# Queries and keys that arrive head dimension first, split for two heads at once, and three small row operations on GpSimd

## What is computed

```python
# q, k, v: [2, 8, 768, 64] float32 (16 heads of 768 tokens), proj: [64, 6]
q_bits = (q @ proj > 0); k_bits = (k @ proj > 0)
q_bucket = sum(q_bits * 2**arange(6)); k_bucket likewise
scores = where(q_bucket[:, None] == k_bucket[None, :], q @ k.T / 8, -1e9)
attn = exp(scores - max(scores)); attn = attn / (sum(attn) + 1e-9)
attn_out = attn @ v            # then x [1536, 512] goes through two mixtures of 8 experts
```

## Time and profile before

| what | value |
|---|---|
| median of three runs | 1698.58 us |
| profiled execution, from first to last instruction | 1694.0 us |
| TensorE, VectorE, ScalarE, GpSimd busy over the span | 94%, 40%, 30%, 18% |
| start of the first exponential | 19.24 us |
| first transposes of attention's output for the expert layer | 304.22 us |
| the same four engines, 150 to 185 us (two heads) | 34.15, 32.91, 28.33, 13.28 of 35.00 us |

### The profile page before, as it was taken

One profiled execution on the slowest core, in us unless ns is written; L12 is line 12 of the kernel. 1 busy time (PEld: TensorE's weight loads), 2 busy tenths in 40 slices (PEclk: granted clock), 3 DMA queues, 4 the chain that ended last, 5 costly groups with the idle time before them and its releaser, 6 DMA issues.

```text
span 1694.0 us, 21627 instructions
## 1 busy us (share of the span) xinstructions
PE 1591.6 (94%) x7588; PEld 1310.1 (77%) x7589; DVE 670.9 (40%) x1227; ACT 505.0 (30%) x943; POOL 309.6 (18%) x381
## 2 busy tenths in 40 slices
PE   7999998789999999999999999999999992699997
PEld 6888887568888888888888888888888871577775
DVE  6999998541211211211221121121122134554324
ACT  5887877301111111111111111111111133643213
POOL 3333341320030030030030030030030004322202
PEclk9999999999999999999999999999999995899999
DMA  5343343110110110020020020010011013753310
GB/s 136 92 119 93 104 124 123 51 50 1 50 50 1 50 50 0 15 84 0 0 99 0 0 99 0 0 65 34 0 50 50 1 50 131 271 176 133 134 43 23
DMA packets 49380, 108.06 MB, mean 64 GB/s; under 512 B 7350, under 2 KB 13494, under 8 KB 49344
## 3 DMA queue, kind: packets, MB, share of 16 engines
q1 hardware_dynamic: 44208, 96.30, 17.3%
q10 hardware_dynamic: 2736, 4.98, 1.0%
q0 software_dynamic: 2400, 6.31, 1.0%
HBM read 81.58 MB, written 13.40 MB: 56 GB/s over the span
## 4 chain that ended last, share of the span: by engine, by line
PE 80%; DVE 7%; issue 5%; ACT 3%; DMA 3%; POOL 2%; DVEq 0%; ACTq 0%; POOLq 0%; SPq 0%
PE psum L353 24%; PE psum L355 23%; PE psum L354 23%; PE psum L576 2%; DVE pt_lo L1069 2%; DMA w_raw<-in_moe_w_dram 2%; DVE row_max L1079 1%; PE psum L528 1%; ACT prob L846 1%; PE psum L784 1%; PE psum L565 1%; ACT pt_hi L839 1%; PE psum L566 1%; PE psum L589 1%; PE psum L590 1%
## 5 line engine op out<-in xcount | busy, mean ns | idle before, releaser
L936 ACT ACTIVATE h_hi<-psum 128x512 fp32r<-128x512 f32 x192 | 114.9, 599 | 871.8 <-PE psum L355 871.8
L353 PE MATMUL psum<-xt_lo,w_hi 128*128 128x512 f32 x768 | 304.8, 397 | 0.0
L355 PE MATMUL psum<-xt_hi,w_lo 128*128 128x512 f32 x768 | 301.6, 393 | 0.0
L353 PE MATMUL psum<-w_lo,h_hi 128*128 128x512 f32 x768 | 299.5, 390 | 1.6 <-issue 1.6
L354 PE MATMUL psum<-xt_hi,w_hi 128*128 128x512 f32 x768 | 299.4, 390 | 0.0
L355 PE MATMUL psum<-w_hi,h_lo 128*128 128x512 f32 x768 | 299.1, 390 | 0.0
L354 PE MATMUL psum<-w_hi,h_hi 128*128 128x512 f32 x768 | 298.8, 389 | 0.0
L1232 DVE SCALAR_TENSOR_TENSOR h_lo<-psum,h_hi 128x512 fp32r<-128x512 f32 x192 | 132.7, 691 | 347.9 <-ACT h_hi L936 347.5
L1262 DVE SCALAR_TENSOR_TENSOR tok<-psum,route,tok 128x512 f32<-128x512 f32 x96 | 65.7, 745 | 436.4 <-PE psum L355 436.4
L379 POOL CAST w_hi<-w_raw 128x512 fp32r<-128x512 f32 x64 | 39.2, 612 | 813.4 <-PE psum L355 813.4
L355 PEld LDWEIGHTS psum<-xt_hi,w_lo 128*128 128x128 f32 x768 | 144.6, 188 | 33.8
(11 more groups left out here) (227 smaller groups left out, 2020.5 us busy)
## 6 DMA issues: line engine op xcount, KB each, us to landing
...
```

The source lines that it names most:

```text
L353: pe.matmul(acc, a[0], b[1], start=start, stop=False)
L355: return pe.matmul(acc, a[1], b[0], start=False, stop=stop)
L936: act.activation(h_s[0][:, f, :], psum[:, f % 4, :], ACT.Relu).then_inc(m1.h_hi, 1)
```

## The change

Queries and keys are laid out otherwise on the host, before the kernel is launched: two heads lie on one another, head dimension first, as [8 pairs, 128, 768]. The kernel loads a pair with two transfers of 384 KB each and splits it into `k_hi`, `k_lo`, `q_hi` and `q_lo` (128 x 768), once for two heads. The transposes of keys and queries and the ScalarE copies behind them are gone. Instead SP moves all six operands of a head from the split tiles, where it moved four before. The hash of half a head has five matmuls: two of them use 64 partitions (`k_lo` against the high and low part of the projection), and one takes both parts of the projection against `k_hi` twice (`proj_mix`). It stands in r1 and r2, one step later than before. The turned outputs are no longer transposed and then added by GpSimd: a float32 matmul with `fold` (two unit matrices on one another, 128x64) turns and adds at once, so that ScalarE copies 192 columns and GpSimd only scales. `row_scale`, `row_bias` and the denominator move from VectorE to GpSimd, which now follows the same steps: row terms of tile g+2 first, then pieces of a split. The reciprocal stays on VectorE, in r1 and r4.

The core of the diff:

```diff
         gate_in = w_gate.rearrange("(k p) e -> p k e", p=P)
+        def load_pair(i):
+
+            sp.wait_ge(s_qk_split, 2 * i)
+            sp.sem_inc(s_load_go, 1)
+            sp.dma_start(k_raw[:], k[i]).then_inc(s_k_in, 16)
+            sp.dma_start(q_raw[:], q[i]).then_inc(s_q_in, 16)
+
...
+        def move(i, u, first=False):
+
+
+            rows = slice(u * D, u * D + D)
+            k_split, q_split, scored = 2 * i + 1, 2 * i + 2, IT * (2 * i + u - 1)
+            sp.wait_ge(s_qk_split, k_split)
+            if not first:
+                sp.sem_inc(s_load_go, 1)
+                sp.wait_ge(s_sc, scored)
+            for dst, src in ((k_hh[u][0:D, :], k_hi), (k_hh[u][D:P, :], k_hi), (k_b[u][0:D, :], k_lo)):
+                sp.dma_start(dst.bitcast(F32), src[rows, :].bitcast(F32)).then_inc(s_moved[u], 16)
+            sp.wait_ge(s_qk_split, q_split)
+            for dst, src in ((q_t[u][0:D, :], q_hi), (q_t[u][D:P, :], q_lo), (q_b[u][0:D, :], q_hi)):
+                sp.dma_start(dst.bitcast(F32), src[rows, :].bitcast(F32)).then_inc(s_moved[u], 16)
+
+        def move_bits(i, u):
+
+            sp.wait_ge(s_bits, 2 * (2 * i + u) + 2)
+            sp.dma_start(k_b[u][HQ:HK, :].bitcast(F32), q_b[u][HK:P, :].bitcast(F32)).then_inc(s_bk[u], 16)
+
+        def pair(i, last=False):
+            move(i, 0)
+            load_v(2 * i + 1, 1)
+            if not last:
+                load_pair(i + 1)
+            move_bits(i, 0)
+            move(i, 1)
+            if not last:
+                load_v(2 * i + 2, 0)
+            move_bits(i, 1)
...
-        load(0, 0)
+        for u in range(2):
+            sp.dma_start(v_raw[u][:].rearrange("p t d -> p (t d)"), v_v[u]).then_inc(s_v_in[u], 16)
+        for u in range(2):
+            sp.wait_ge(s_k_b, u + 1)
+            move(0, u, first=True)
+        load_pair(1)
         sp.dma_start(gate_raw[:], gate_in).then_inc(s_setup_dma, 16)
         sp.dma_start(one_col[:, 0:1], tau.partition_broadcast(P)).then_inc(s_setup_dma, 16)
...
+        move_bits(0, 0)
+        load_v(2, 0)
+        move_bits(0, 1)
+        sp.wait_ge(s_zeros, 1)
+        with sp.Fori(1, NH // 2 - 1) as it:
+            pair(it)
+            fill(it - 1)
+        pair(NH // 2 - 1, last=True)
+        fill(NH // 2 - 2)
...
+        def split_qk(i, r):
+
+            if r == 0:
+                pool.wait_ge(s_moved[1], 96 * i)
+                pool.wait_ge(s_k_in, 16 * i + 16)
+                copy(k_hi[:], k_raw[:]).then_inc(s_qk_hi, 1)
+            if r in (1, 2):
+                a = slice((r - 1) * HALF, r * HALF)
+                pool.wait_ge(s_qk_hi, 2 * i + 1)
+                sub = pool.tensor_tensor(k_lo[:, a], k_raw[:, a], k_hi[:, a].bitcast(F32), ALU.subtract)
+                if r == 2:
+                    sub.then_inc(s_qk_split, 1)
+                    pool.wait_ge(s_q_in, 16 * i + 16)
+                    copy(q_hi[:], q_raw[:]).then_inc(s_qk_hi, 1)
+            if r == 3:
+                pool.wait_ge(s_qk_hi, 2 * i + 2)
+                pool.tensor_tensor(q_lo[:], q_raw[:], q_hi[:].bitcast(F32), ALU.subtract).then_inc(s_qk_split, 1)
...
+        def row_terms(it, u, t):
+
+            g = IT * (2 * it + u) + t
+            c = slice(t % 2, t % 2 + 1)
+            pool.wait_ge(s_max, g + 1)
+            pool.sem_inc(s_pool_go, 1)
+            pool.tensor_scalar(row_scale[:, c], row_max[:, c], -BIG / 2, SCALE, ALU.is_gt, ALU.mult).then_inc(s_scale, 1)
+            pool.wait_ge(s_scale, g + 1)
+            pool.sem_inc(s_pool_go, 1)
+            pool.tensor_scalar(row_bias[:, c], row_max[:, c], row_scale[:, c], -1.0, ALU.mult,
+                               ALU.mult).then_inc(s_bias, 1)
+
...
+        def step(it, kk):
+            g = 2 * IT * it + kk
+            if known(it, g + 2):
+                row_terms(*at_step(it, kk, 2))
+            if kk % 3 == 0 and known(it, g - 3):
+                i, u, t = at_step(it, kk, -3)
+                denominators(i, u, t // 3)
+            if kk % 3 == 1 and known(it, g - 7):
+                i, u, t = at_step(it, kk, -7)
+                tail(i, u, t // 3)
+            i, r = divmod(kk, 2 * IT)
+            if r < 4 and known(it, 2 * IT * (it + i + 1)):
+                split_qk(it + i + 1, r)
+            if kk % IT == IT - 1 and known(it, g + 1):
+                i, u = divmod(kk // IT + 1, 2)
+                split_v(it + i, u, first=isinstance(g, int) and g < IT)
...
-                    mm = pe.matmul(psum[:, bank, 0:HALF], w[part][:], src[:, half * HALF:(half + 1) * HALF],
-                                   start=(w is proj_w[0] and part == 1), stop=(w is proj_w[1] and part == 0))
+            a = slice(half * HALF, (half + 1) * HALF)
+            o = psum[:, bank, 0:HALF]
+            if half == 0:
+                pe.wait_ge(s_moved[u], 96 * it + 96)
+            for part in (1, 0):
+                pe.matmul(o, proj_w[0][part][:], q_t[u][:, a], start=(part == 1), stop=False)
+                pe.matmul(o, proj_w[1][part][0:D, :], k_b[u][0:D, a], start=False, stop=False)
+            mm = pe.matmul(o, proj_mix[:], k_hh[u][:, a], start=False, stop=True)
             mm.then_inc(s_proj, 1)
...
-                tr = pe.transpose(psum[:, 7, j * P:(j + 1) * P], o_t[:, j * P:(j + 1) * P], ident[:])
-            tr.then_inc(s_o_nat, 1)
+                mm = pe.matmul(psum[:, 7, j * D:(j + 1) * D], o_t[:, j * P:(j + 1) * P], fold[:], start=True, stop=True)
+            mm.then_inc(s_o_nat, 1)
...
-                    pe.wait_ge(*((s_qk_ready, 4 * n + 8) if kk % IT == 0 else (s_bits, 2 * n + 4)))
+                pe.wait_ge(s_bits, 2 * (n + kk % IT // 3) + 2 if known(it, IT * (n + kk % IT // 3)) else 2 * NH)
                 turn_outputs(it, kk)
...
+        for part in range(2):
+            rows = slice(part * D, part * D + D)
+            link(dve.tensor_copy(proj_mix[rows, :], proj_w[1][part][rows, :].bitcast(F32)))
...
-        dve.wait_ge(s_raw[0], 48)
-        for rows, raw in ((k_s[0], k_raw[0]), (q_s[0], q_raw[0])):
-            link(dve.tensor_copy(rows[:, :, 0:D].bitcast(F32R), raw[:]))
-            dve.tensor_tensor(rows[:, :, D:2 * D].bitcast(F32R), raw[:], rows[:, :, 0:D],
-                              ALU.subtract).then_inc(s_qk_split, 1)
+        dve.wait_ge(s_k_in, 16)
+        dve.tensor_copy(k_hi[:], k_raw[:]).then_inc(s_qk_hi, 1)
+        dve.wait_ge(s_qk_hi, 2)
+        dve.tensor_tensor(k_lo[:], k_raw[:], k_hi[:].bitcast(F32), ALU.subtract).then_inc(s_qk_split, 1)
+        dve.tensor_tensor(q_lo[:], q_raw[:], q_hi[:].bitcast(F32), ALU.subtract).then_inc(s_qk_split, 1)
...
-            dve.wait_ge(s_max, g + 1)
-
-            dve.tensor_scalar(row_scale[:, c], row_max[:, c], -BIG / 2, SCALE, ALU.is_gt, ALU.mult).then_inc(s_scale, 1)
-            dve.wait_ge(s_scale, g + 1)
-            dve.scalar_tensor_tensor(row_bias[:, c], row_max[:, c], -1.0, row_scale[:, c], ALU.mult,
-                                     ALU.mult).then_inc(s_bias, 1)
...
+        a = inputs[name]
+        if name in ("q", "k"):
+            nb, nh, ns, nd = a.shape
+            a = a.reshape(nb * nh // 2, 2, 128, ns // 128, nd).transpose(0, 1, 4, 3, 2).reshape(nb * nh // 2, 2 * nd, ns)
+        a = _np.ascontiguousarray(a)
```

211 lines of the change are left out of this document (60 added, 151 removed).

## The result

The changed kernel takes 1723.35 us (median of 4 runs, 1720.17 to 1729.55); the kernel before 1697.53 (4 runs, 1694.59 to 1700.28). The ratio is 1.016, with a 95% interval of 1.0135 to 1.0184: 1.6% slower, where 1699 us and a range up to 1715 were forecast. The profiled execution has a span of 1718.5 us against 1694.0, so the traces have to account for 24.5 us.

The account below looks back on a forecast made before the run. Three close chains were taken to bound attention: TensorE's work, late VectorE, and an `exp` latency chain setting a 2.5 us step floor. Terms +8.0 - 7.0 + 0.5 - 1.2 = +0.3 us gave 1699 us, range 1685 to 1715.

Parts of the forecast that it names:

- The step that failed: Hash in r1 and r2: five matmuls a half at 0.17 us each, no extra for 64 partitions, each step 2.91 us.
- forecast -6.5 and +0.5: Attention heads: -6.5 us over heads 1 to 13; +0.5 for the last two, which pay for fifth matmul and folds.
- Rival C: Slower through transfers: prologue +10, late hashes, or 64-partition matmuls costing 0.05 each (+2 +5); 1706 us, chance 0.16.
- Before the first head, +8.0: Program start: key bits queue behind moves and loads, 3.2 MB in all, landing at 24.8 not 16.76; bounds +5 to +10.
- r0 and r3, 3.1 us: Output-turning steps: 0.7 to start, 0.98 for the six-pass fold, 0.2 copy, 1.24 from `exp` to next step.
- r3, "no stall, but no slack": Fold in r3: second-half hash bits ready 3.6 us after r2 starts, 0.7 after r3 starts, so no wait.
- r4 and r5, 2.5 us: Steps without key and query transposes: r4 stays at 2.5 and r5 falls from 2.98, bound by the `exp` latency chain.
- rival B: Slower: GpSimd row terms above 0.3 us per operation delay the bias past `exp`; at 0.5 us +14, 1713; chance 0.16.
- VectorE's relief "not counted again": VectorE loses two small operations a step and the denominators; this lets steps fall as forecast, with no separate gain.
- SP "nothing, with little cover": Moves and loads grow from 1.5 to 1.9 MB per head; landing at about 11 us, wanted at 12.5; no cost.
- End of attention, -1.2: Last chain: one GpSimd operation goes (1.39 us and 0.07), the fold adds 0.45, the copy gives back 0.2.
- forecast as -0.5 us each: Steady heads: steps sum to 17.0 us against 17.5 per head, -7.0 us over 14 heads.

Follow-up runs that it names:

- group64: Changed kernel with the two 64-partition hash matmuls of a half side by side at the end; ratio to the kernel before 1.0088.
- rows128: Changed kernel with zero rows in the weights making all five hash matmuls of a half 128 partitions high; ratio to the kernel before 1.0057.
- before64: Kernel before with its key hash matmuls cut to 64 partitions, leaving the keys' low parts out; ratio to the kernel before 1.0141.
- best4: nofold with the first head loaded directly without moves except its key bits, and four hash matmuls per half; ratio to the kernel before 0.9955.
- rows128_dve: rows128 with row scale and row bias put back on VectorE, denominators staying on GpSimd; ratio to the kernel before 1.0098.
- halves: rows128 with projection loads first, first key bits moved ahead of the second head's operands, and `q_lo` cut in two; ratio to the kernel before 1.0036.
- nofold: rows128 with projection loads first, first key bits moved ahead of the second head's operands, and the fold undone; ratio to the kernel before 1.0000.

## Why the prediction was wrong, step by step

- **The step that failed:** "Two of the five use 64 partitions, which no row shows; [...] so I take no extra, with 0.05 us per matmul around these". They cost 0.8 us a half: r1 is 0.87 and r2 0.81 over the forecast, 23.5 us over heads 1 to 14. That is nearly the whole miss of the heads (forecast -6.5 and +0.5, measured +15.3 and +1.9, 23.2 apart); the errors of the other steps (r0 -0.18, r3 -0.08, r5 +0.21) nearly cancel. Shown by group64, rows128 and, from the other side, before64. The bound was no bound: it came from rows in which nothing changed height. A mode that the trace does not hold cannot be bounded by matmuls of another mode. Rival C named the place, with 5 us for it; C as a whole had the chance 0.16.
- **Before the first head, +8.0:** measured +11.4, and the step that was to set it did not. The forecast let the key bits wait behind 3.2 MB in the queue until 24.8. In the changed kernel they waited for the hash: the first head's moves had landed at 18.10 (216 GB/s between 12 and 18 us, where the earlier trace rows show 237), the ten hash matmuls, which I had not priced because the queue seemed longer, take 5.9 us, and the bits' move then takes 2.2: they are there at some 26.9, 2.1 us late. The other 1.3 us come behind that: the scores run at a pitch of 0.32 us (26.98 to 28.67, for 16.89 to 17.86 before: 0.7), and the row terms of the first tile stand bare on GpSimd (the first `exp` 1.97 us after the row maximum begins, for 1.38: 0.6). Splitting started at 8.66 as forecast (8.7), but by luck: the projection was there at 5.31 and not at 6.4, while VectorE's small operations took 3.2 us and not 2.2, two of them 0.42 and 0.84 us long beside a GpSimd operation. Rival C's +10 was nearer.
- **r0 and r3, 3.1 us:** 2.92 and 3.02. The fold starts 0.72 us into the step (forecast 0.7). Its six passes take 0.58 (160.91 to 161.49), 0.10 each and not the 0.13 of the earlier trace rows; by this the Trainium skill's price of a weight load ("TensorE: Matmul & The Clock Gate", LDWEIGHTS), columns/1.2 ns, an estimated 0.107 us for 128 columns, was the better one. I took the single row of a kernel's other phase, where the pair's pitch could not be read from starts.
- **r3, "no stall, but no slack":** no stall in the changed kernel, because r2 was long; a stall of 0.18 us as soon as r2 has the forecast's length (rows128), 0.27 in best4. The bits are there 3.65 us after the start of r2 (forecast 3.6); the 0.20 us from there to the fold were not counted.
- **r4 and r5, 2.5 us:** r4 2.49. r5 2.57 in odd heads and 2.88 in even ones, the small form of rival B: GpSimd's operation takes 0.23 and 0.27 us rather than 0.18, and a handover 0.2 rather than 0.07, so the slack of 0.3 us is gone and `q_lo` in front adds 0.30.
- **VectorE's relief "not counted again":** right in the sum, wrong in place: it works through the bits in r3 (rows128_dve, +0.54 per head if undone).
- **SP "nothing, with little cover":** right; halves showed how little.
- **End of attention, -1.2:** measured -1.4.
- The net of the change without the height changes, in the heads, was forecast as -0.5 us each. It is -0.25 with the fold (rows128) and -0.57 without it (nofold).
